# The addition to the attention's row sums, moved from ScalarE to GpSimd

## The reference

```
scores = q @ k.T / sqrt(64) - slope[h] * |rel|         # only 0 <= rel < 128, else -1e9
attn = exp(scores - scores.max(-1))
attn = attn / (attn.sum(-1) + 1e-9)                    # the 1e-9 is the addition spoken of here
x = attn @ v                                           # then (2304, 512)
h = relu(x @ w1[e]); out += p[:, e] * (h @ w2[e])      # 4 experts, F = 1024
```

## Time and profile before

| | |
|---|---|
| median of 3 runs | 986.52 us (985.45 to 987.59) |
| the profiled execution | 986.28 us, of which the span is 984.4 us |
| PE busy | 953.0 us (97%) |
| POOL busy | 637.9 us (65%), 570 instructions |
| DVE busy | 567.0 us (58%), 1097 instructions |
| ACT busy | 463.9 us (47%), 1022 instructions |
| the chain that ended last | PE 82%, POOL 4%, issue 3%, DVE 3%, ACT 3% |

### The profile page before, as it was taken

One profiled execution on the slowest core, in us unless ns is written; L12 is line 12 of the kernel. 1 busy time (PEld: TensorE's weight loads), 2 busy tenths in 40 slices (PEclk: granted clock), 3 DMA queues, 4 the chain that ended last, 5 costly groups with the idle time before them and its releaser, 6 DMA issues.

```text
span 984.4 us, 18544 instructions
## 1 busy us (share of the span) xinstructions
PE 953.0 (97%) x6077; PEld 790.7 (80%) x6077; DVE 567.0 (58%) x1097; ACT 463.9 (47%) x1022; POOL 637.9 (65%) x570
## 2 busy tenths in 40 slices
PE   8899999999999999999999999999999999999896
PEld 5578888888888888888888888878889989897532
DVE  4645565565565685665565565755665656555602
ACT  5776544544544664444454454554344444332312
POOL 4786667567669797666666677896867666651000
PEclk9899999999999999999999999999999999999998
DMA  8634314213213223223223221127212222137896
GB/s 255 189 94 133 90 44 131 89 54 121 89 64 112 90 65 112 91 68 107 89 78 97 89 86 44 47 87 298 86 43 85 65 63 85 44 125 284 339 381 239
DMA packets 86404, 116.92 MB, mean 119 GB/s; under 512 B 6208, under 2 KB 56896, under 8 KB 86352
## 3 DMA queue, kind: packets, MB, share of 16 engines
q1 hardware_dynamic: 84736, 109.89, 34.3%
q0 software_dynamic: 1616, 6.36, 1.6%
HBM read 111.51 MB, written 4.72 MB: 118 GB/s over the span
## 4 chain that ended last, share of the span: by engine, by line
PE 82%; POOL 4%; issue 3%; DVE 3%; ACT 3%; DMA 1%; DVEq 0%; POOLq 0%; ACTq 0%; SPq 0%
PE banks L1435 37%; PE banks L1416 31%; PE banks L1359 3%; PE banks L1311 2%; PE banks L1572 1%; PE banks L1599 1%; POOL h_lo L688 1%; PE banks L1333 1%; DVE w_lo L1098 1%; PE banks L1380 1%; ACT pr L796 1%; PE banks L1335 1%; POOL ws_lo L679 1%; DMA out<-slot_w 1%; PE banks L1498 1%
## 5 line engine op out<-in xcount | busy, mean ns | idle before, releaser
L1126 DVE SCALAR_TENSOR_TENSOR acc<-banks,prob,acc 128x512 f32<-128x512 f32 x288 | 215.4, 748 | 194.0 <-PE banks L1435 193.8
L1435 PE MATMUL banks<-w_hi,h_lo 128*128 128x512 f32 x576 | 228.8, 397 | 0.0
L1435 PE MATMUL banks<-w_hi,h_hi 128*128 128x512 f32 x576 | 226.5, 393 | 1.8 <-POOL h_lo L688 1.8
L1435 PE MATMUL banks<-w_lo,h_hi 128*128 128x512 f32 x576 | 227.9, 396 | 0.0
L688 POOL TENSOR_TENSOR h_lo<-c,h_hi 128x384 fp32r<-128x384 f32 x141 | 147.5, 1062 | 104.9 <-ACT c L883 104.8
L881 ACT ACTIVATE h_hi<-c 128x384 fp32r<-128x384 f32 x141 | 73.1, 518 | 152.3 <-PE banks L1435 95.8
L679 POOL TENSOR_TENSOR ws_lo<-w_sum,ws_hi 128x1024 fp32r<-128x1024 f32 x47 | 115.5, 2457 | 42.0 <-ACT ws_hi L857 41.9
L1416 PE MATMUL banks<-xT_hi,ws_hi 128*128 128x384 f32 x376 | 128.5, 342 | 1.5 <-POOL ws_lo L679 1.5
L1435 PEld LDWEIGHTS banks<-w_hi,h_lo 128*128 128x128 f32 x576 | 108.3, 188 | 23.1
L1416 PE MATMUL banks<-xT_lo,ws_hi 128*128 128x384 f32 x376 | 126.5, 336 | 0.0
L1416 PE MATMUL banks<-xT_hi,ws_lo 128*128 128x384 f32 x376 | 126.1, 335 | 0.0
(11 more groups left out here) (176 smaller groups left out, 1601.8 us busy)
## 6 DMA issues: line engine op xcount, KB each, us to landing
w_raw<-w SPq DMA_DIRECT2D x96, 512.0 KB, 4.1
slot_w<-m2w SPq DMA_DIRECT2D x4, 2048.0 KB, 11.7
v_b<-v_n SPq DMA_DIRECT2D x24, 256.0 KB, 5.3
slot_early<-m2w POOLq DMA_DIRECT2D x3, 2048.0 KB, 13.4
slot_early<-m2w SPq DMA_DIRECT2D x3, 2048.0 KB, 11.4
v_a<-v_n SPq DMA_DIRECT2D x20, 256.0 KB, 5.4
out<-slot_w SPq DMA_DIRECT2D x9, 512.0 KB, 4.5
q_b<-q_t SPq DMA_DIRECT2D x12, 288.0 KB, 4.7
```

What stands on the lines that cost most here:

```text
L1126: dve.scalar_tensor_tensor(acc[:, tile, :], ps_y[tt % 2][:, :], prob[:, tile, bass.ds(e, 1)], acc[:, tile, :], ALU.mult, ALU.add).then_inc ...
L1435: ins = pe.matmul(ps_y[tt % 2][:, :], hh[:, f, tt * P:(tt + 1) * P], wp[u % 2][:, f, :], start=m == 0, stop=m == 3 * FT - 1)
```

## The change

ScalarE no longer adds 1e-9 to the row sums. GpSimd does, with an instruction of its own on 128x2 elements. In the lead its place is at v, for step v+4, ahead of the normalisation of step v+3. In the body it stands two pieces after the step's beginning, the same piece at which VectorE's inverse stands, and one before the normalisation. VectorE's inverse waits for the same semaphore as before, which GpSimd now raises. ScalarE's own wait for its exponentials goes too.

```diff
-            for s_x in (s_norm, s_lop):
+            for s_x in (s_norm, s_lop, s_rplus):
                 pool.sem_inc(s_x, FROM)
...
+            def row_sums(p, n, a, lead):
+                pool.wait_ge(s_exp, FROM + place(n, a) + 1)
+                if not lead:
+                    pool.nop(nofuse=True)
+                pool.tensor_scalar(rsum[:, a, :], rsum[:, a, :], 1e-9, None, ALU.add).then_inc(s_rplus, 1)
+
...
+                j = v + LEAD_I
+                if 0 <= j < LEAD:
+                    row_sums(*step(j), True)
                 j = v + LEAD_N
                 if 0 <= j < LEAD:
                     norm(*step(j), True)
...
+                        for s_ in body_steps(p, e, last, [b + 2 for b in BODY_S], t):
+                            row_sums(*s_, False)
                         for s_ in body_steps(p, e, last, [b + 3 for b in BODY_S], t):
                             norm(*s_, False)
...
-            for s_x in (s_exp, s_oc, s_rplus):
+            for s_x in (s_exp, s_oc):
                 act.sem_inc(s_x, FROM)
...
                 ins.then_inc(s_exp, 1)
-                act.wait_ge(s_exp, FROM + place(n, a) + 1)
-                act.activation(rsum[:, a, :], rsum[:, a, :], ACT.Copy, bias=1e-9).then_inc(s_rplus, 1)
```

## The result

The changed kernel takes 996.32 us (median of 4 runs, 996.09 to 997.3), the kernel before on the same chip 985.99 (4 runs, 985.26 to 987.59; the 986.52 that I started from was the median of three of them): 1.0105 times as long, 95% interval 1.0089 to 1.0121. It is 10.3 us slower, where I forecast 4.4 (990.9 us, range 987.5 to 995.0). The sign was right, the size less than half. The profiled execution took 997.3 us, of which the span is 995.5; it is the slowest of the four runs, 1.0 us above their median.

What follows compares the result with a forecast made beforehand. TensorE bounds the body; in the lead GpSimd's queue is fullest. Lead 1.7 plus passage 2.7 make 4.4 us over 986.28: 990.7, given as 990.9 us; own range 989 to 993, 8-in-10 range 987.5 to 995.

Steps and rivals of the forecast that it cites:

- Ordinary steps of the body: Body outside the passage: GpSimd adds before VectorE reaches the inverse, 1.0 us of cover for a 0.3 us chain; no loss.
- ScalarE's gain: Lead, steps 20 to 26: 0.24 us a step, 1.7 us at most, lost to waiting for VectorE's minima; body nothing.
- The first rival: Lead stays ScalarE's: its 1.7 us show at the lead's end, the passage costs nothing, 984.8 us; chance 0.08.
- The price of an addition: On GpSimd, 0.13 us from start to start for 128x2, between 0.04 (fills) and 0.61 (a normalisation).
- Lead, 29 to 41 us: GpSimd's split of w1 delayed, step 13's inverse and next minima about 2 us late, mostly absorbed: 0.2 us late.
- Lead, 42 to 63 us: GpSimd's queue without pause makes step 23's inverse 3.5 us late; TensorE starts 1.5 us late and stays so.
- the early lead: The lead's stretch from 29 to 41 us, taken as 0.2 us late.
- The clock: New pauses near 54 and 364 us bring another low-clock stretch: 1.7 to 3.4 us more, about 993.4; chance 0.20.
- Passage: Body, first pass to second, GpSimd without pause from 333 to 363 us: steps 48, 49 and 50 lose 2.7 us.
- Step 50: Passage: addition behind the weight sums makes VectorE's split of h late; TensorE's product 1.7 us late.
- Step 48: Passage: addition behind the sums of x gives TensorE a 0.4 us pause, swallowed by its own 0.56 at 351.29: 0.
- the far price of an addition: Upper end for 8 additions on the lead's path: 8 x 0.48 = 3.8 us more, 994.7 us.

Runs made afterwards that it cites:

- no_passage: Kernel before, with GpSimd making the body's additions except those of steps 48 to 50, ScalarE the rest: 985.44 us (1.0006).
- no_add: Kernel before with the addition of 1e-9 left out altogether, VectorE's inverse waiting for the exponentials: 985.03 us (0.9998).
- tt_add: Changed kernel with the addition in two-tensor form, a tensor of 1e-9 in place of the constant: 992.86 us (1.0083).
- price: Kernel before plus 72 spare additions with a constant on GpSimd, waiting for nothing and awaited by nobody: 989.76 us (1.0045).
- unwaited: Kernel before plus 72 spare GpSimd additions, each waiting for its step's exponentials; VectorE's inverse still waits for ScalarE alone: 993.79 us (1.0093).
- early: Changed kernel with additions moved ahead of long works in GpSimd's queue, in lead and passage: 994.17 us (1.0093).
- norm_first: Changed kernel with the lead's normalisation of step v+3 put ahead of the addition of step v+4: 996.74 us (1.0123).
- lead_only: Kernel before with GpSimd making only the lead's 27 additions, ScalarE keeping the body's 45: 991.17 us (1.0061).

## Why the prediction was right or wrong

**Ordinary steps of the body: 0.** Right (0.2 of the trace, no_passage 1.0006). The second and fifth step of each six, which I named as the closest, come out with no cover left, for a reason that I had not seen:

```profile
134.67 1.02 POOL L694 TENSOR_TENSOR h_lo<-c,h_hi 128x384 fp32r<-128x384 f32 x1 [1.62 <-ACT c L892]
135.77 1.07 POOL L652 TENSOR_SCALAR rsum<-rsum 128x2 f32<-128x2 f32 x1
```

The addition takes 1.07 us while VectorE runs its split of w2 (134.96 + 1.81 = 136.77), and the inverse starts at 136.94, 0.18 after VectorE was free. The Trainium skill (SBUF — State Buffer, Who interferes with whom) has the two engines hold the shared port in turn for whole instructions; the trace agrees, as the addition ends at 136.84, 0.07 behind the split. Of the three steps that I had passed over with "without anything of TensorE's behind them", step 46 costs 0.5.

**ScalarE's gain is lost.** Right; no_add shows nothing to be had (985.03 against 985.05). The first rival falls with it.

**The price of an addition: 0.13.** Wrong, and one of the two large errors. It measures 0.42 in this form. I took it from the eight fills of 128x1, "nearest in elements": but those are eight of a kind in a row, and here each stands alone between instructions of another form. My outer bound of 0.61 had held it; I should have stayed nearer to the middle of 0.04 and 0.61, as nothing in the trace spoke for the fills but their size. The sign that I had set for it, an addition more than 0.3 us from the next start, was badly chosen: that distance is 0.29, and the other 0.13 stand ahead of the addition, where the overlap with the one before is lost. By the prediction's own count (8 on the path) the step to 0.42 is 8 x 0.29 = 2.3 us. tt_add bears this out: at 0.15 an addition, near the forecast, it loses 1.8 us from step 17 to step 27, where I had 1.5.

**Lead, 29 to 41 us: 0.2.** Wrong: 1.9 + 0.9. The inverse of step 13 was late by 2.1 us, as worked out, but "the exponentials there waited for ScalarE, which takes most of it" was not so: with ScalarE relieved and VectorE stuck the next minima were what exponentials waited for, and step 15 came 1.9 late. price and unwaited, which differ in GpSimd's wait alone (0.6 and 2.7 us lost by step 17), show that this wait, ahead of the split, is enough to start a loss of this size. The 0.9 is the port's order turned round, in no term of the sum. This loss does not hang on the price: tt_add has 2.1 of it by step 17. early did not cure it either; there the wait only moved to the inverse of step 14. What the 0.9 is worth by itself no run shows: norm_first, where VectorE's split takes 1.20 us, loses 0.7 from step 16 to step 17 all the same.

**Lead, 42 to 63 us: 1.5.** The mechanism is as told: no pause of GpSimd from 44 to 66 us, the inverse of step 23 behind it, TensorE's wait for a normalisation, of 2.34 us at 57.27. The size is not: from step 17 to step 27 the trace has 5.4 us, of which the clock has 1.5 and 3.9 are left (4.0 in lead_only), and 1.5 + 2.3 for the price is 3.8. I put the sums of x at 43.43 and the inverse of step 23 at 58.26; they were at 45.03 and 61.14. The 1.6 of the first are the early lead; the rest is five additions at 0.42 instead of 0.13. And I let VectorE's slack behind the inverse swallow 1.7 of 3.5 us, which it can do once: with GpSimd's queue as the bound, each further normalisation came late by the whole.

**The clock (a rival, 0.20).** It occurred, with less than I gave it and, as far as the traces show, in the profiled execution alone: 1.5 us, where TensorE is full, and nothing in the 13.7 us, where VectorE's late minima and then GpSimd's queue were the bound.

**Passage: 2.7.** The steps in their order were 0, 1.0 and 1.7; they measure 0.8, 1.4 and 1.9, with 0.5 from step 46. Step 50 is right in place and size. Step 48 failed in "TensorE's own pause at 351.29 swallows it": that pause was for GpSimd's low part of h, and GpSimd is itself late by what it waits for. GpSimd after:

```profile
344.92 0.21 POOL L652 TENSOR_SCALAR rsum<-rsum 128x2 f32<-128x2 f32 x1
345.49 0.83 POOL L658 TENSOR_TENSOR pr<-pr,rinv 128x384 f32<-128x384 f32 x1 [0.35 <-DVE rinv L1075]
346.28 1.46 POOL L669 TENSOR_TENSOR w_sum<-w_raw 128x256 f32<-128x256 f32 x1
```

The normalisation stands straight behind its own step's addition, so GpSimd gives a result away and waits 0.35 us for the answer: 0.08 + 0.21 + 0.35 = 0.65 us a step in a queue without a pause, and the weight sum behind it takes 1.46 instead of 0.74, as VectorE's split of x now falls on it (345.97 + 1.16). Against this the second pair of the sums of x takes 2.10 instead of 2.71, as I had forecast. I had charged GpSimd only with the addition.

**The sum.** Lead 1.7 forecast, 6.3 measured alone; passage 2.7 against 4.5. The steps that failed are the price of an addition (0.13, measured 0.42) and the early lead (0.2, measured 2.8), and with less weight step 48 (0, measured 0.8). TensorE's pauses stand about where they were forecast (a normalisation at 57.27, forecast 53 to 55; 362.56 and 373.63, which less the 7 us of the lead are 355.6 and 366.6), only longer. The range ended at 995.0; it had the far price of an addition in it (3.8), and the clock's case, but never both beside a wrong early lead.

## What to carry to other kernels

A tiny instruction put into a queue without a pause costs the distance between the starts of its neighbours, not its span, and that distance depends on what stands beside it; bound it by the nearest row of the same form between the same neighbours, and where there is none keep the whole range. A result handed to another engine and read back by the next instruction of the same queue costs the queue a round trip as well (0.65 us here, for 0.21 of work). A wait put ahead of a long piece of work puts that work off, and with it all that stands behind it or shares its port (2.1 us by step 17 here). And a pause of the bound engine swallows a delay only if the work it waits for is not on the engine that is being delayed.

## What the runs showed of the hardware

- On GpSimd an addition of 128x2 with a constant, between instructions of two tensors, has a span of 0.21 us and costs 0.42; with a second tensor in place of the constant its span is 0.19 to 0.20 and it costs 0.15. The Trainium skill (Perfetto Trace Analysis, GPSIMD Engine Instruction) advises to read starts of neighbours in place of spans; the two forms, with nearly equal spans and prices of 0.42 and 0.15, bear it out.
- An addition of 256 numbers on GpSimd takes 1.07 us (12 times in the changed kernel's trace) while VectorE runs an operation of two SBUF tensors, and VectorE's own split goes from 1.20 to 1.80 us when GpSimd's normalisation starts 0.10 ahead of it.
- Where GpSimd's split of w1 and VectorE's split of x met, the one that started first kept its time and the other waited: VectorE 1.04 and GpSimd 3.07 (instead of 2.36) with VectorE 0.19 ahead; GpSimd 2.35 and VectorE 3.11 (instead of 0.96) with GpSimd 0.06 ahead.
- Full clock in place of half from 36 to 48 us left the start of GpSimd's sums of x where it was (45.20 against 45.03), as other engines were the bound. A stretch of 3.4 us at half clock in which TensorE was full cost 1.5.
